# Small copies move to ScalarE, one pass's meetings move a step, loads and buffers change places

## Time and profile before

| | us |
|---|---|
| median of 3 runs | 948.69 |
| lowest and highest of them | 948.62, 950.83 |
| the profiled execution | 946.26 |
| its span, first to last instruction | 944.5 |

### The profile page before, as it was taken

How to read it: one execution, slowest core, us unless ns; L and a number is a source line. 1 busy time by engine, 2 the same in 40 slices (tenths; PEclk the granted TensorE clock), 3 DMA queues, 4 the chain that set the end, 5 groups by cost and what they waited for, 6 DMA issues and landing times.

```text
span 944.5 us, 17521 instructions
## 1 busy us (share of the span) xinstructions
PE 922.5 (98%) x7062; PEld 768.8 (81%) x7062; DVE 536.8 (57%) x778; ACT 358.2 (38%) x760; POOL 303.8 (32%) x246
## 2 busy tenths in 40 slices
PE   6799999999999999999999999999999999999998
PEld 6789888888888888888788888888888888888887
DVE  7898986667666766213874553463473373364332
ACT  4456554444444445335464123123223223213212
POOL 6688654545454544323451011011001001101000
PEclk9999999999999999999999999999999999999999
DMA  9864442233223321004321000010000001000000
GB/s 245 250 180 127 115 115 75 60 88 103 75 59 105 80 73 50 21 5 151 93 68 67 1 34 34 1 34 33 1 34 34 1 8 61 0 1 34 1 1 33
DMA packets 32943, 60.19 MB, mean 64 GB/s; under 512 B 6112, under 2 KB 19936, under 8 KB 32864
## 3 DMA queue, kind: packets, MB, share of 16 engines
q1 hardware_dynamic: 27152, 50.89, 18.6%
q10 hardware_dynamic: 5712, 8.20, 3.0%
HBM read 47.46 MB, written 9.44 MB: 60 GB/s over the span
## 4 chain that ended last, share of the span: by engine, by line
PE 86%; DVE 6%; ACT 3%; issue 2%; DMA 1%; POOL 1%; SPq 0%; ACTq 0%; DVEq 0%; POOLq 0%
PE acc L1053 32%; PE bank L1037 11%; PE bank L1039 11%; PE bank L1038 11%; PE pair L1038 5%; PE pair L1037 5%; PE pair L1039 5%; DVE cum L690 2%; DVE ki L707 1%; PE pair L1106 1%; DVE ki L714 1%; ACT att L500 1%; PE pair L1135 1%; PE pair L1164 1%; DMA x<-x_dram 1%
## 5 line engine op out<-in xcount | busy, mean ns | idle before, releaser
L1053 PE MATMUL acc<-gs,w_dn 128*128 128x512 f32 (+1 forms) x1512 | 357.5, 382 | 0.7 <-POOL gs L930 0.7
L1053 PEld LDWEIGHTS acc<-gs,w_dn 128*128 128x128 f32 x1512 | 272.8, 188 | 55.7 <-POOL gs L930 1.5
L930 POOL TENSOR_TENSOR gs<-act_g,gs 128x512 fp32r<-128x512 f32 (+1 forms) x96 | 122.3, 1274 | 203.6 <-ACT gs L534 203.4
L1037 PE MATMUL bank<-xs,w_up 128*128 128x512 f32 (+1 forms) x480 | 180.1, 375 | 6.5 <-POOL w_up L917 2.3
L1039 PE MATMUL bank<-xs,w_up 128*128 128x512 f32 (+1 forms) x480 | 176.6, 368 | 0.0
L1038 PE MATMUL bank<-xs,w_up 128*128 128x512 f32 (+1 forms) x480 | 176.6, 368 | 0.0
L777 DVE SCALAR_TENSOR_TENSOR act_g<-act_u,bank 128x512 f32<-128x512 f32 (+1 forms) x112 | 68.0, 607 | 133.1 <-ACT act_u L526 132.4
L847 DVE TENSOR_TENSOR act_u<-act_u,bank 128x512 f32<-128x512 f32 x72 | 49.5, 688 | 149.1 <-ACT act_u L594 149.1
L526 ACT ACTIVATE act_u<-bank,half 128x512 f32<-128x512 f32 (+1 forms) x112 | 70.0, 625 | 136.2 <-PE bank L1039 136.1
L1037 PEld LDWEIGHTS bank<-xs,w_up 128*128 128x128 f32 x480 | 90.3, 188 | 25.3 <-DVE state L738 3.7
L598 ACT ACTIVATE gs<-act_g 128x512 fp32r<-128x512 f32 x72 | 45.5, 632 | 157.7 <-DVE act_g L853 157.7
(11 more groups left out here) (119 smaller groups left out, 1113.9 us busy)
## 6 DMA issues: line engine op xcount, KB each, us to landing
rkn<-in_rkN SPq DMA_DIRECT2D x22, 384.0 KB, 4.1
rkt<-in_rkT SPq DMA_DIRECT2D x44, 192.0 KB, 3.6
val<-in_valN SPq DMA_DIRECT2D x22, 256.0 KB, 2.9
dec<-in_decT SPq DMA_DIRECT2D x48, 97.5 KB, 2.7
x<-x_dram SPq DMA_DIRECT2D x6, 768.0 KB, 4.3
x_dram<-xo SPq DMA_DIRECT2D x5, 768.0 KB, 4.2
out<-xo SPq DMA_DIRECT2D x5, 768.0 KB, 3.2
raw_dn<-in_w_out SPq DMA_DIRECT2D x14, 192.0 KB, 4.9
```

The costliest lines, as they stand in the source:

```text
L930: pool.tensor_tensor(gs[:, f % GRING, 1, tok], act_g[:, f % 2, tok], gs[:, f % GRING, 0, tok].bitcast(F32), ALU.subtract).then_inc(s_glo, 1)
L1037: pe.matmul(dst, w_hi, x_hi, start=first, stop=False)
L1053: last = pe.matmul(ps_o[m][:, tok], w[:, wp, m * P:(m + 1) * P], gs[:, f % GRING, xp, tok], start=f == 0 and a == 0, stop=f == nf - 1 and ...
```

## The change

- `keep_last` goes from VectorE (behind `prep_scan` in PREP) to ScalarE (at the head of INV1, before `copy_keys`); `prep_scan` now waits until the last columns of group g-2 were copied.
- `sum_bonus` goes from INV1 into PREP, between `scale_state` and `prep_k`. In pass 0 that of group 2 goes from step 1 to step 0.
- `half_a`: every phase of pass 0 is one step later. The sums of groups 1 to 3 use the other PSUM bank of the hidden slices.
- ScalarE issues the first loads of r, k and `u_h` behind its first activation (which brings its table load) and not before it; VectorE sets `half`, on which that activation waits, first.
- SyncE issues `load_x2(0)` ahead of `store_x2(PASSES - 2)`, not behind it.
- SBUF: `raw`, `act_u`, `act_g`, `xo`, `rms_s`, `half` and `ones` move behind the attention's tiles, with a `gap` of 5792 bytes so that they share no byte with these. `xs` then starts at 98304, `gs` at 122880, the attention's tiles and after them `w_x` at 139264, `raw` at 192160.

```diff
-        raw = sb("raw", [P, SRING, KT * P])
         xs = sb("xs", [P, 2, 2, KT, TT], F32R)
-        act_u = sb("act_u", [P, 2, TT])
-        act_g = sb("act_g", [P, 2, TT])
         gs = sb("gs", [P, GRING, 2, TT], F32R)
-        xo = sb("xo", [P, KT, TT])
...
+        gap = sb("gap", [P, 1448])
+
+        raw = sb("raw", [P, SRING, KT * P])
+        act_u = sb("act_u", [P, 2, TT])
+        act_g = sb("act_g", [P, 2, TT])
+        xo = sb("xo", [P, KT, TT])
...
-            return ps_o[2] if g == 0 else ps_h[0]
+            return ps_o[2] if g == 0 else ps_h[g < B]
...
-        half_a = {3: [(MEET, 1)], 5: [(PREP, 1)], 6: [(INV1, 1), (INV2, 1)],
-                  7: [(MEET, 2)], 8: [(PREP, 2)], 9: [(INV1, 2)], 10: [(INV2, 2)],
-                  11: [(MEET, 3)], 12: [(PREP, 3)], 13: [(INV1, 3)]}
+        half_a = {4: [(MEET, 1)], 6: [(PREP, 1)], 7: [(INV1, 1), (INV2, 1)],
+                  8: [(MEET, 2)], 9: [(PREP, 2)], 10: [(INV1, 2)], 11: [(INV2, 2)],
+                  12: [(MEET, 3)], 13: [(PREP, 3)], 14: [(INV1, 3)]}
...
-            store_x2(PASSES - 2)
...
             load_x2(0)
+            store_x2(PASSES - 2)
             store_x2(PASSES - 1)
...
+            def keep_last(g):
+
+                act.wait_ge(s_cum, g + 1)
+                act.activation(last[0:DP, g % LASTS, :], cum[0:DP, slot(g), :, :, T:T1].rearrange("p a b t -> p (a b t)"),
+                               ACT.Copy).then_inc(s_last, 1)
...
+                if phase == INV1 and g + 3 < GROUPS:
+                    keep_last(g + 3)
                 if phase == INV1 and has_state(g + 1):
                     copy_keys(g + 1)
...
+            act.wait_ge(s_half, 1)
+            act.activation(y3[:, 0, 0:1], half[:, :], ACT.Copy)
             for g in range(2):
                 for j in (1, 0):
...
-            act.wait_ge(s_half, 1)
-            act.activation(y3[:, 0, 0:1], half[:, :], ACT.Copy)
...
+            for g in range(2):
+                keep_last(g)
             split_up(0)
...
+                if f in (1, 4):
+                    keep_last((2, 3)[f // 4])
...
+                need(dve, s_last, g - 1)
                 dve.tensor_tensor_scan(
...
                     if g + 2 < GROUPS:
+                        sum_bonus(g + 2)
                         prep_k(g + 2)
                     if g + 3 < GROUPS:
                         prep_scan(g + 3)
-                        keep_last(g + 3)
-                if phase == INV1 and g + 2 < GROUPS:
-                    sum_bonus(g + 2)
...
+                if f == 0:
+                    sum_bonus(2)
                 if f < 2:
                     prep_inv(2, f)
-                if f == 1:
-                    sum_bonus(2)
                 if f == 2:
                     prep_k(2)
+                if f == 3:
+                    prep_scan(3)
                 for phase, g in half_a.get(f, ()):
                     attention(phase, g, 0)
-                if f == 3:
-                    prep_scan(3)
-                    keep_last(3)
-                    prep_inv(3, 0)
-                if f == 4:
-                    prep_inv(3, 1)
+                if f in (4, 5):
+                    prep_inv(3, f - 4)
```

More of the change, by code:

```diff
@@ L82, in build @@
         w_dn = sb("w_dn", [P, NF1, 2, DM], F32R)
-        raw = sb("raw", [P, SRING, KT * P])
         xs = sb("xs", [P, 2, 2, KT, TT], F32R)
-        act_u = sb("act_u", [P, 2, TT])
-        act_g = sb("act_g", [P, 2, TT])
         gs = sb("gs", [P, GRING, 2, TT], F32R)
-        xo = sb("xo", [P, KT, TT])
-        rms_s = sb("rms_s", [P, KT])
-        half = sb("half", [P, 1])
-        ones = sb("ones", [P, P], F32R)
         attn_mem = ExitStack()
@@ L121, in build @@
         last = sa("last", [P, LASTS, PAIRS * PB])
-        rk_t = [xo[:, g, :].rearrange("p (a t) -> p a t", a=PAIRS) for g in range(PLACED)]
         upper = att[:, 0, 0, 0:2, :].rearrange("p a t -> p (a t)")
@@ L131, in build @@
         nt = sb("nt", [P, TT])
+        gap = sb("gap", [P, 1448])
[3 more added lines that the diff above has]
+        xo = sb("xo", [P, KT, TT])
+        rms_s = sb("rms_s", [P, KT])
+        half = sb("half", [P, 1])
+        ones = sb("ones", [P, P], F32R)
+        rk_t = [xo[:, g, :].rearrange("p (a t) -> p a t", a=PAIRS) for g in range(PLACED)]
         ps_h = [ctx.enter_context(nc.psum_tensor(f"bank{i}", [P, 512], F32)) for i in range(2)]
@@ L692, in prep_scan @@
                                        ALU.mult, ALU.add).then_inc(s_cum, 1)
-            def keep_last(g):
-                dve.wait_ge(s_cum, g + 1)
-                dve.tensor_copy(last[0:DP, g % LASTS, :], cum[0:DP, slot(g), :, :, T:T1].rearrange("p a b t -> p (a b t)")).then_inc(s_last, 1)
             def prep_inv(g, part):
@@ L858, in tile2 @@
                                       gs[:, f % GRING, 0, :].bitcast(F32), ALU.subtract).then_inc(s_hlo, 1)
+            dve.memset(half[:, :], 0.5).then_inc(s_half, 1)
             for q in range(2):
@@ L863, in _ @@
             dve.memset(first1[:, :, :, 0:1], 1.0).then_inc(s_first1, 1)
-            dve.memset(half[:, :], 0.5).then_inc(s_half, 1)
             dve.wait_ge(s_first1, 2)
@@ L875, in _ @@
             for g in range(2):
-                keep_last(g)
-            for g in range(2):
                 x1_lo(g, 0)
@@ L880, in _ @@
             prep_scan(2)
-            keep_last(2)
             for f in range(NF1):
                 hidden(0, f)
+                if f == 0:
+                    sum_bonus(2)
                 if f < 2:
                     prep_inv(2, f)
-                if f == 1:
-                    sum_bonus(2)
                 if f == 2:
                     prep_k(2)
+                if f == 3:
+                    prep_scan(3)
                 for phase, g in half_a.get(f, ()):
                     attention(phase, g, 0)
-                if f == 3:
-                    prep_scan(3)
-                    keep_last(3)
-                    prep_inv(3, 0)
-                if f == 4:
-                    prep_inv(3, 1)
+                if f in (4, 5):
+                    prep_inv(3, f - 4)
             run1(1, cycles(1), 1)
```

## The result

On one chip the changed kernel took 937.66 us (median of 4 executions, 936.33 to 938.1) and the kernel before 949.76 (4 executions, 948.62 to 953.06): a ratio of 0.9865 [0.9836, 0.9893]. Measured again it was 936.77 (5 executions) against 951.11 (11), 0.985 [0.9823, 0.9877].

The account below looks back on a forecast made before the run. The prediction took TensorE, 86% of the chain of waits, as the bound, through its idle time and pitch. Terms -0.3 - 3.9 + 1.0 - 2.6 - 3.2 = -9.0 us took the median from 948.69 to 939.7; range 937.2 to 945.0.

Parts of the forecast that it names:

- the layout term: Blocks with `w_x`: moving it to 139264, a multiple of 64 and lower, restores the usual matmul pitch, -3.2 us.
- Head, -0.3 forecast: Before the first `up`: r and k issued behind the table load let the decays land sooner, -0.3 us.
- r and k start when `half` is set, some 0.3 us later: Head: the table load does not hold issuing, so r and k go out only some 0.3 us later.
- Pass 0, -3.9 forecast: First `up` to fourth MEET: later meetings, earlier sums and moved copies cut TensorE's idle time, -3.9 us.
- the bound of -4.8: Pass 0's largest gain: all of TensorE's idle time goes except the wait for L917, -4.8 us.
- Of 6.3 us idle, 1.5 stay with the third weight slice (GpSimd, L917) and 0.8 here: Pass 0: TensorE keeps waiting 1.5 us for GpSimd's weights and `sums` 0.8 us at the third meeting; -3.9 us.
- Pass 1, +1.0 forecast: Pass 1: moved sums lengthen VectorE's part and may wait for GpSimd, against the copy saved; +1.0 us.
- the 0.47: Pass 1: sums moved ahead of the gate lengthen VectorE's part by 0.47 us; the time freed behind is unused.
- I take 0.5: Pass 1: the sums' new wait for GpSimd's product in one group, up to 0.9 us, taken as 0.5.
- x2, -2.6 forecast: Pass 6: x2's load issued ahead of the store arrives before ScalarE's square, ending its stall; -2.6 us.
- A slow `w_x`: Rival: `w_x` blocks stay slow at the new place, 942.9 us; chance 0.27.
- ScalarE as the bound: Rival: ScalarE bounds passes 0 and 1, losing their -2.9 us; 942.6, or 945.8 with slow `w_x`; chance 0.14.

Follow-up runs that it names:

- head_only: Kernel before with only the head's edit (`half` set first, table load ahead of r and k): 950.26 us against 949.77, ratio 1.0.
- attention_only: Kernel before with `keep_last` on ScalarE, sums first and pass 0 meetings one step later; old head, load order, layout: 940.71 us, ratio 0.9916.
- single edits: Kernel before with one attention edit each: `keep_last` on ScalarE, sums first, or later meetings; first `up` to pass 1 took 50.31, 48.63, 47.93 us.
- place_only: Kernel before with only the changed SBUF layout: 948.1 us against 951.82, ratio 0.9964.
- after: The changed kernel with all edits, in its first profiled execution: 937.9 us; median 937.66 against 949.76 for the kernel before.
- changed_again: The changed kernel run again without an edit: 936.77 us against 951.11 for the kernel before.

## Why the prediction was wrong

The direction was right, and so was most of what was to happen in pass 0 and to x2; pass 1 went the other way, the layout term came true for a wrong reason, and the clock was left out. Read at equal start and equal clock, the sum in the traces is -4.6 - 0.8 - 2.7 - 3.2 = -11.3 us. The mean clock of 0.9948 against 0.9921 (13 executions and 43), at the 0.7 us for each 0.001 given below, is an estimated -1.9 on top: -13.2, and the medians say -12.1 and -14.3. A direct pair bears this out: `head_only` and the changed kernel both stopped in `outputs` and both fell to half clock in the head, and their spans are 948.2 and 936.2.

- **Head, -0.3 forecast, 0 measured.** The step that failed is "r and k start when `half` is set, some 0.3 us later": they started 0.17 later. That moved nothing in the DMA queue, and the decays landed as before. The reading that issuing is not held by a table load was right, and the Trainium skill (ScalarE: Activation LUTs, What ACT_TABLE_LOAD costs) has its 1.28 us of load here too, with no drain of 1.38 us behind it: the activation follows at 2.10 where the load ends at 2.09.
- **Pass 0, -3.9 forecast, -4.6 measured at equal start.** The trace of `attention_only` has -5.8, which looks past the bound of -4.8; 1.2 of it is L917's wait, shorter because the first `up` came 1.03 later. The waits for the scores, 2.23, and for the state, 1.4, went as the working had it. The step that failed is "Of 6.3 us idle, 1.5 stay with the third weight slice (GpSimd, L917) and 0.8 here". The earlier trace rows have 2.3 for L917, in two places, of which the working kept only the longer; and 2.3 is no fixed amount either, it is 1.1 at a first `up` of 21.68 to 21.95 and nothing in the 13 profiles with one at 22.02 or later, where TensorE also starts at half clock. `sums`, the 0.8, waits 0.2. The gain of single edits, set right for the clock, gives no sign that the three do more together than apart.
- **Pass 1, +1.0 forecast, -0.7 to -0.8 measured. This is the largest miss, 1.8 us.** The single edits seem to bear out most prices: the copy -0.87 forecast and -0.86 measured, the sums +1.9 and +1.25, the wait for GpSimd up to 0.9 and 0.91. But `place_only` took 1.1 us more in this pass with neither moved, so the +1.25 of one profile is no measure of the sums. The step that failed is to add "the 0.47" and "I take 0.5" to durations left as they were. They are not fixed: scaling 0.55 to 1.40, key product 1.51 to 1.03, scan 2.05 to 1.77 in this group. Gate to gate all this came to +0.05, where the sum had +0.55 (0.47 for the sums, 0.5 for the wait, less 0.42 for the copy). What the runs show in its place is that the new order takes the same time however the tie of the two engines ends: 4.79 us gate to gate with the scaling at 1.40 (`after`), which then covers the wait for GpSimd, and 4.92 with the scaling at 0.55 and the wait (`attention_only`), where the old order has 4.74 or 5.79. The prediction took the kernel before in its better case.
- **x2, -2.6 forecast, -2.7 measured.** Load at 416.70, by 418 as forecast, no wait at the square, and seven steps in 29.07 where 29.1 was said. The chain in order of time, against the earlier trace rows:
```profile
421.99 2.04 PE acc L1055 x9
...
451.06 2.04 PE acc L1055 x9
```
  The timeline of SyncE and ScalarE, against the earlier trace rows:
```profile
416.70 0.33 SPq L449 DMA_DIRECT2D x<-x_dram  x1
...
432.28 1.48 ACT L559 ACTIVATE ntmp<-x 128x1536 f32<-128x1536 f32 x1
```
- **Layout, -3.2 forecast, -3.2 measured; right for a wrong reason.** The timeline of TensorE, against the earlier trace rows:
```profile
489.65 0.39 PE L1039 MATMUL bank<-xs,w_x 128*128 128x512 f32 x1
...
510.05 0.39 PE L1039 MATMUL bank<-xs,w_up 128*128 128x512 f32 x1
```
- **Rivals.** A slow `w_x` and ScalarE as the bound did not happen: the copy takes 0.2 us there, and waits for the scan where nothing needed it. The groups by line (busy us, mean ns of one | idle time before), against the earlier trace rows:
```profile
L723 DVE TENSOR_TENSOR ki<-rkt,ki 112x512 f32<-112x512 f32 x24 | 34.2, 1424 | 0.2
...
L507 ACT ACTIVATE last<-cum 112x8 f32<-112x8 f32 x24 | 4.8, 202 | 6.5 <-DVE cum L704 6.5
```
  The copies went from 18.3 us on VectorE to 4.8 on ScalarE. The key products grew from 21.7 to 34.2 us in the same trace, nearly as much as VectorE gave away, and TensorE had no wait for them behind pass 1.

By parts, the medians of kernels with one part each are 0.0 for the head [-2.2, +2.1], -8.0 for the attention edits [-11.2, -4.8], -4.2 for x2 [-6.1, -2.2] and -3.4 for the layout [-5.0, -1.8] (each ratio, less 1, times about 950): -15.6 us, against -12.1 and -14.3 for all of them. Each part is above its trace's term (-5.4, -2.7, -3.2), within its interval, and the falls of the clock spared by fewer stalls would do this for the first two; for the layout nothing of the kind is shown.

## What to carry to other kernels

Compare two profiles only after taking off what is not the edit's: the start of the stretch and its time at half clock. Here single edits seemed to give 3.1 us and the three together 5.8, and with both set right they are an estimated 5.2 and 4.6. Read more than one execution before a number is taken as the kernel's own: the one with a clock of 1.000 was 3.5 us faster than the median and had the earliest first `up` of 17, by up to 4.4 us. Where two engines that slow each other start within some 20 ns, treat both outcomes as possible and prefer an order of instructions that costs the same in either. And lay weights and moving operand out at the same place of a 256-byte period; a buffer of odd size between them cost 1 to 3% of each matmul, and six to ten matmuls behind them were slow too.

## What was not expected of the hardware

- The granted clock of one kernel varies between executions: 0.987 to 0.996 in 43 of the kernel before, with times from 946.98 to 955.08, some 0.7 us for each 0.001 by a line through them (`head_only`: 946.46 at 1.000, 953.92 at 0.987). In 16 of the 17 profiled executions it falls to the 1.2 GHz level between 13.0 and 20.7 us, behind stretches in which TensorE was busy 2.1 to 2.7 of 4 us in the three looked at (`after`, `head_only`, `changed_again`), and is back at 20.8 to 30.9. In the profiled execution of before it was as little busy (2.71, 2.30, 3.12 of 4) and the clock stayed; what decides is open. Later falls, before the end, came at 31 to 37 us in four and at 455 to 460 us in four of the kernels that kept the old meeting steps or the old order of x2, and in none of the eight with both new.
- In eleven of 17 profiled executions TensorE stops once for 1.7 to 2.9 us in `outputs`, and the other engines with it. In these the trace's first packets of instruction fetch in this stretch come at 18.3 to 19.2 us and not at about 15.5. Whether the fetch is the cause was not tried.
- VectorE's instructions take up to several times as long by what GpSimd does beside them: in the profile of before the copy of 112x8 from 0.15 us with nothing beside it to 0.99, the scaling of the state 0.55 or 0.96, and 1.40 in the one after, the key product 0.68 to 1.51. A start 16 ns behind GpSimd's product instead of 13 makes the scaling 0.85 us longer and the product 0.4 us shorter.
- TensorE's pace for 512 columns is 226.7 ns with weights and moving operand 0 or 256 bytes apart, 233.4 with the weights 64 bytes further on, 232.6 with 128, 229.5 with the moving operand 64 bytes further on; and it stays slow for six to ten matmuls behind such a stretch.
